# The normaliser of an mLSTM output: multiplied into the output bank by VectorE instead of into the gate by GpSimd

## The reference, cut to what matters

```python
for t in range(S):
    m_new = np.maximum(f_gate[:, :, t] + m, i_gate[:, :, t])
    ...
    C = f_stab[:, :, None, None] * C + i_stab[:, :, None, None] * np.einsum('bhd,bhe->bhde', vt, kt)
    n = f_stab[:, :, None] * n + i_stab[:, :, None] * kt
    h_tilde = np.einsum('bhde,bhe->bhd', C, qt)
    nq = np.einsum('bhd,bhd->bh', n, qt)[:, :, None]
    denom = np.maximum(np.abs(nq), 1.0)
    o = 1.0 / (1.0 + np.exp(-o_gate[:, :, t]))
    y[:, :, t] = o * h_tilde / denom
...
h = x @ w_in;  g = np.maximum(0.01 * h, h);  x = g @ w_out     # first MLP
h = x @ w_in;  g = h * np.cos(h);            out = g @ w_out   # second MLP
```

## Time and profile before

| | |
|---|---|
| median of 3 runs | 846.08 us (845.98 to 847.89) |
| the profiled execution's own time | 848.12 us |
| its span | 846.2 us |
| PE busy | 819.8 us (97%) |
| DVE busy | 623.8 us (74%), 1346 instructions |
| ACT busy | 466.6 us (55%) |
| POOL busy | 341.1 us (40%), 352 instructions |
| L1270, POOL, gate by `nrm` | 24 times, median 723 ns |
| L1041, DVE, bank by gate | 44 times on `s` banks, median 314 ns |
| granted TensorE clock, mean | 0.984 |

### The profile page before, as it was taken

How to read it: one execution, slowest core, us unless ns; L and a number is a source line. 1 busy time by engine, 2 the same in 40 slices (tenths; PEclk the granted TensorE clock), 3 DMA queues, 4 the chain that set the end, 5 groups by cost and what they waited for, 6 DMA issues and landing times.

```text
span 846.2 us, 18185 instructions
## 1 busy us (share of the span) xinstructions
PE 819.8 (97%) x6908; PEld 788.3 (93%) x6908; DVE 623.8 (74%) x1346; ACT 466.6 (55%) x1050; POOL 341.1 (40%) x352
## 2 busy tenths in 40 slices
PE   6889899999999999999999999999999999999997
PEld 5788899999999999999999999999999999999997
DVE  5668667776677776776763488888888888888886
ACT  5234443343433433334336677767776777677776
POOL 4745643343343333343304653333333333333332
PEclk9589999999999999999999999999999999999999
DMA  9455634422323433225004320302020202010000
GB/s 249 127 166 160 172 92 127 131 81 78 124 78 107 136 110 126 78 77 192 1 31 136 119 110 1 118 1 70 1 72 1 71 1 70 1 62 10 11 14 24
DMA packets 37971, 70.57 MB, mean 83 GB/s; under 512 B 3584, under 2 KB 25088, under 8 KB 37888
## 3 DMA queue, kind: packets, MB, share of 16 engines
q1 hardware_dynamic: 37840, 69.40, 26.5%
q10 hardware_dynamic: 48, 0.05, 0.0%
HBM read 57.44 MB, written 11.99 MB: 82 GB/s over the span
## 4 chain that ended last, share of the span: by engine, by line
PE 83%; DVE 7%; issue 4%; ACT 3%; DMA 2%; POOL 1%; SPq 0%; DVEq 0%; POOLq 0%; ACTq 0%
PE h L593 30%; PE acc L605 12%; PE acc L607 11%; PE acc L606 11%; PE s L593 10%; DVE kvo_s L991 2%; PE s L535 2%; PE s L551 2%; PE s L563 2%; PE x L571 1%; DVE D L999 1%; ACT g_hi L728 1%; DMA e_dram<-r_f 1%; ACT kvo_s L728 1%; PE acc L671 1%
## 5 line engine op out<-in xcount | busy, mean ns | idle before, releaser
L593 PE MATMUL h<-xT,w_in 128*128 128x384 f32 x1536 | 306.8, 341 | 0.2 <-DVE w_in L1170 0.2
L593 PEld LDWEIGHTS h<-xT,w_in 128*128 128x128 f32 x1536 | 266.6, 188 | 3.3 <-DVE w_in L1170 0.5
L728 ACT ACTIVATE t_f<-h 128x384 f32<-128x384 f32 x192 | 94.1, 490 | 296.8 <-PE h L593 296.7
L605 PE MATMUL acc<-w_out,g_hi 128*128 128x320 f32 x768 | 241.7, 315 | 2.2 <-POOL g_lo L1412 1.8
L607 PE MATMUL acc<-w_out,g_lo 128*128 128x320 f32 x768 | 237.3, 309 | 0.0
L606 PE MATMUL acc<-w_out,g_hi 128*128 128x320 f32 x768 | 235.9, 307 | 0.0
L1412 POOL TENSOR_TENSOR g_lo<-g_f,g_hi 128x384 fp32r<-128x384 f32 x127 | 130.0, 1024 | 212.1 <-ACT g_hi L728 212.1
L1096 DVE TENSOR_TENSOR g_f<-h,t_f 128x384 f32<-128x384 f32 x128 | 71.2, 556 | 112.3 <-ACT t_f L728 112.2
L605 PEld LDWEIGHTS acc<-w_out,g_hi 128*128 128x128 f32 x768 | 144.2, 188 | 4.6 <-POOL g_lo L1412 1.9
L606 PEld LDWEIGHTS acc<-w_out,g_hi 128*128 128x128 f32 x768 | 144.4, 188 | 0.0
L607 PEld LDWEIGHTS acc<-w_out,g_lo 128*128 128x128 f32 x768 | 144.1, 188 | 0.0
(11 more groups left out here) (139 smaller groups left out, 803.4 us busy)
## 6 DMA issues: line engine op xcount, KB each, us to landing
qk_s<-qk SPq DMA_DIRECT2D x24, 512.0 KB, 3.8
kvo_s<-kvo SPq DMA_DIRECT2D x24, 484.0 KB, 5.8
x_dram<-stage SPq DMA_DIRECT2D x8, 960.0 KB, 6.0
xT<-x_dram SPq DMA_DIRECT2D x8, 960.0 KB, 4.9
D<-g_dram SPq DMA_DIRECT2D x42, 128.0 KB
qe<-q SPq DMA_DIRECT2D x24, 160.0 KB, 4.2
eG_b<-e_dram SPq DMA_DIRECT2D x48, 80.0 KB
out<-x SPq DMA_DIRECT2D x24, 160.0 KB, 1.8
```

The costliest lines, as they stand in the source:

```text
L593: last = nc.tensor.matmul(bank[:, 0:BLOCK], w(a), x[:, k, :], start=(n == 0), stop=(n == 7))
L605: nc.tensor.matmul(acc[t][:, 0:DM], g_hi[:, s, r], w_out[:, 0, j, :], start=(j == 0), stop=False)
L728: copy = lambda o, i, **k: nc.scalar.activation(o, i, ACT.Copy, **k)
```

## The change

`gated` is gone from POOL. DVE multiplies each of the two output banks in place by its half of `nrm`, directly behind the reciprocal in `normaliser`: two instructions more per unit, 48 in all, and one wait on its own semaphore. `outputs` then waits for DVE's own products and for the sigmoid in place of POOL. Nothing is moved on PE, ACT and SP.

```diff
@@ normaliser(b, c)
                 nc.vector.reciprocal(nrm[:, p, :], nrm[:, p, :]).then_inc(nrm_done, 1)
+                dve.wait_ge(nrm_done, n + 1)
+                for e, x in enumerate(parts):
+                    o = output_heads(b, c, e)[:, :, 0:HD]
+                    last = tt(o, o, x.unsqueeze(2).to_broadcast([P, SIDE, HD]), ALU.mult)
+                last.then_inc(normed_done, 1)
@@ outputs(b, c)
-                dve.wait_ge(gated_done, unit(b, c) + 1)
+                dve.wait_ge(normed_done, unit(b, c) + 1)
+                dve.wait_ge(sig_done, unit(b, c) + 1)
@@ POOL
-            def gated(b, c):
-
-                pool.wait_ge(nrm_done, unit(b, c) + 1)
-                pool.wait_ge(sig_done, unit(b, c) + 1)
-                o = o_s[:, c % BUFS, :].rearrange("p (h d) -> p h d", h=HEADS)
-                nc.gpsimd.tensor_tensor(o, o, nrm[:, c % 2, :].unsqueeze(2).to_broadcast([P, HEADS, HD]), ALU.mult).then_inc(gated_done, 1)
@@ unit_masks(b, c)
                 own_state(b, c)
-                gated(b, c)
@@ POOL's prologue
             first_keys(2)
-            gated(0, 0)
             first_scaled(2)
             own_state(0, 2)
-            gated(0, 1)
             split_in_lo(0)
             second_inputs()
-            gated(0, 2)
             second_columns()
```

More of the change, by code:

```diff
@@ L186, in build @@
         nrm_done = sem("nrm_done")
-        gated_done = sem("gated_done")
+        normed_done = sem("normed_done")
         ph_done = sem("ph_done")
```

## The result

The change makes the kernel faster, by half a per cent.

| | median of this | median of before | ratio, 95% interval |
|---|---|---|---|
| first | 841.9 us (841.07 to 844.13, 6 runs) | 846.84 us (845.98 to 847.89, 6 runs) | 0.9950 [0.9936, 0.9964] |
| once more, beside other kernels | 842.94 us (841.97 to 844.16, 8 runs) | 846.12 us (844.67 to 848.78, 13 runs) | 0.9962 [0.9949, 0.9975] |

The account below looks back on a forecast made before the run. PE, 97% busy, was taken as the bound, so only its idle time and clock count. 848.12 - 4.6 (prologue) + 5.5 (loop) = 849.0 profiled; medians lie 2.04 lower, so 847.0 us, range 843.2 to 850.6.

Parts of the forecast that it names:

- rival 1: Loop: no loss, as POOL's instructions come later or their collision hits nothing; prologue still gives 4.6; 841.5 us, chance 0.13.
- the block: Loop: POOL's four instructions for the next unit, to start when `Cm` ends, 2.9 us earlier than before.
- the collision: Loop: READ's `g_lo` meets POOL's running line 1245 and ends 0.57 us late, in 12 units.
- The new DVE work: All units: 48 DVE instructions, 0.55 us per pair, fitting into idle time or under warm-ups, so costing nothing.
- The prologue's chain: Prologue: POOL no longer waits for the third unit's normaliser, so PE's transposes begin 2.40 us earlier, at 40.87.
- The clock in the prologue: Prologue: PE idle only 1.0 us, so its clock stays at 2.4 GHz; gain 4.6 us, or 2.4 if lost.
- The loop's loss: Loop: READ's `g_lo`, held by POOL, delays `x1` and PE in 12 units by 0.46 each, 5.5 us lost.
- Lateness: Loop, READ: `g_lo` ends at 138.44 instead of 137.87, so `outputs` and `x1` are 0.57 us late.
- Slack: Loop: of the gap between `x1`'s end and PE's weight load, 0.10 us is left before PE waits.
- The lower bound of the sum: Loop: if POOL's first instruction is not held, the loss is 12 x 0.14 = 1.7 us.

Follow-up runs that it names:

- kernel with the block held late: The full change plus a POOL wait for DVE's two products, so the next unit's four POOL instructions start where they did before; 842.02 us, ratio 0.9953.
- one-line move: The kernel before, with POOL's gate of the third unit moved behind the two instructions of second_columns, no DVE product added; 842.90 us, ratio 0.9958.

## Why the prediction was wrong

**The sign and the sum.** Forecast 847.0, 0.9 slower; measured 841.9, below the range. The sum had two terms, 4.6 gained and 5.5 lost. The first came out somewhat smaller, 3.7 in the mean of the traces; the second was too large by a factor of 5 to 10, with 0.6 to 1.1. Together that is 2.6 to 3.1 us faster, at the lower end of what the two comparisons of medians give, 3.2 and 4.9. The number is nearest to rival 1, 841.5, but not its mechanism: the block did come early and the collision did hit. That its 841.5 lies so close to the measured 841.9 is in part luck: the gain of 4.6 that it has is too large, and so is its loss of nothing too small.

**The new DVE work: right.** 0.56 per pair against 0.55, in idle time of which 0.77 is left. The kernel with the block held late has all 48 products and the fastest loop of the kernels with the change in their loop.

**The prologue's chain: right.** 2.38 against 2.40 where PE's clock stood as in before. That it was POOL's order, not its work, is shown by the one-line move.

**The clock in the prologue: right where its condition held.** The forecast took it that PE would be idle for 1.0 us. That needed the transposes of the second unit at 38.75, bound by warm-ups at the low clock. In five of the seven new prologues the clock rose sooner; the transposes of the second unit ran at 0.49, PE came to them early and then stood idle for 2.4 us and more, since POOL and DVE were the bound again, and the clock fell all the same; slot 0's product took 2.05 to 2.79. In the two others it took 1.66 and 1.68. So 2.4 to 4.6 was the honest term, and the mean is 3.7. Neither trace with the old prologue kept the clock: slot 0's product took 2.91 and 2.73. The moment at which the clock rises is not the kernel's alone: one code had it up at 27 us in one execution and at 37 in another. The Trainium skill (TensorE: Matmul & The Clock Gate, "What's actually happening") says that the gate's window runs freely and isn't reset when a kernel starts. The traces agree in that the moment varies; they do not show by what.

**The loop's loss: the step that failed.** It is the term of 12 units times 0.46, 5.5 us. Everything up to a late `x1` came as said: the block began behind `Cm`, READ's `g_lo` was held in a dozen units, TURN's no more. Then three sizes were wrong.
- Lateness, 0.57 forecast, 0.38 measured. I let the waiting `g_lo` of OUTPUTS go ahead of POOL's first instruction, as at 53.66. Here POOL went first: `g_lo` took 1.70 and line 1241 its plain 1.06. So the block ended 4.50 behind `Cm`, not 4.70. That `g_lo` did not mind, as it had the idle time behind it. The row that I took was of another case: at 53.00 `g_lo` had begun 0.70 us before POOL's running instruction ended, in the loop 0.20 to 0.29.
- Slack, 0.10 forecast, 0.20 to 0.22 measured. I read it off PE's weight load. The load is issued ahead of its matmul; when it begins to wait, the product in front is still streaming: in the unit above it ends at 131.08 (129.50 + 1.58), and the late load came at 131.04.
- What the moved block gives back, taken as nothing. At the passage between batches READ's `g_lo` was held before as well, 0.95, and now took 0.69; the passage fell from 20.39 to 20.19, twice. And in the last unit of a block of three, the next transposes of PE had waited for DVE's `x_lo`, which stood behind the TURN slot's long `g_lo`. With that `g_lo` at 0.55 the row is gone from the waits, 75 to 442 us. In before it reads (us in total, times, longest):

```profile
PEld x L571 <- DVE xT L1075: 1.0, 3, 0.3
```

Passage by passage, after against before: nine of the twelve units pay 0.14 to 0.27 each, 1.7 together; the three that are last in their block pay nothing (0.01, -0.09 and -0.09); two passages between batches give back 0.2 each. That makes the 1.1 of the stretches, and 0.6 against an execution with the lost race. That the three units pay nothing because of the missing wait fits the rows and was not tested alone. The lower bound of the sum, 1.7 with POOL's first instruction not held, had the right order of the two engines and still the slack of 0.10; the measured loss lies below it. The price was multiplied by 12, and its two largest parts were each taken from a row that was one step away from what it should have measured.

**Left open.** Which of two waiting instructions goes first. In the twelve traces a `g_lo` that had begun 0.30 us or more before POOL's running instruction ended went ahead of POOL's next one, 24 times of 24; with less than that, POOL's went first 42 times of 54. What decides is not shown. Open is also whether more warm-ups keep the clock in the prologue; the one execution fell into the wrong case for it.

No version beats the change beyond the noise. The kernels at 842.0 to 842.9 differ by less than their runs do; the one-line move gets there with the least.

## What to carry to other kernels

When a multiplication leaves an engine, look at what stood in line behind the wait that it had: here one move in POOL's order was worth the gain as far as the medians can tell, and the engine that took the work over had no part in it. Slack ahead of TensorE is not the gap before the weight load: measure it by adding work of a known size and look where the line of prices starts. Two instructions that start within 0.01 us of each other make a race, and one trace shows only one of its ends: here that was 0.4 us, where the price to be measured was 1.1. And a loss of a few hundredths per unit that is multiplied by a dozen must be taken from rows of the same place, or carried with both of its ends.

## What the runs showed of the hardware

- VectorE's 128x160 product from PSUM into the same PSUM bank took 0.56 us for two, the same as into SBUF (0.55).
- A VectorE instruction with two SBUF inputs that met a running GpSimd instruction could be passed over by the next one: `g_lo` took 1.70 us, and ended 0.41 behind GpSimd's second instruction (125.36 + 1.06 = 126.42, end 126.83). Where the two started within 0.01 us of each other, the one that was first took its plain time: with VectorE first GpSimd's took 1.69 instead of 1.29, with GpSimd first VectorE's took 1.69 instead of 0.55.
- Behind a product of eight matmuls TensorE took an operand 0.20 to 0.22 us late for nothing, where the row of the weight load showed a gap of 0.10. In the change, at 0.38 late, that row showed a wait of 0.28 and the unit paid some 0.2.
- The granted clock reached its upper level at 27 us in one execution and at 37 in another of the same code, and fell again after idle stretches of 2.4 us and more, not after one of 0.71.
